# Turned answers first at a pair's end, and weight splitting one pair later between the answers, in a recurrence with two MLPs on one core

## The chip, the cores and the metric

One core of one Trainium2 chip. The metric is the device time of one launch in microseconds (us), lower is better. The engines are TensorE (PE, its weight loads are PEld), VectorE (DVE), ScalarE (ACT), GpSimd (POOL) and SyncE (SP), whose queue issues nearly all DMAs. Each runs its own instruction stream in order and waits on semaphores.

## The reference

```python
B, H, S, D = 4, 8, 768, 40
for t in range(S):                               # recurrence, a D x D state per head
    y[:, :, t] = einsum('bhd,bhde->bhe', r[t], state)
    Sa = einsum('bhde,bhe->bhd', state, a[t])
    state = state * w[t][:, :, None, :] - outer(Sa, b[t]) + outer(v[t], k[t])
x = y as (3072 tokens, 320)
h = x @ w_in;  x = (h - tanh(h)) @ w_out          # first MLP, 320 -> 2048 -> 320
p = domain_probs / (domain_probs.sum(-1) + 1e-9)
out = sum over e < 4 of p[:, e] * (relu(x @ w1[e]) @ w2[e])   # experts, 320 -> 1024 -> 320
```

## The kernel before

**Tiling.** The recurrence is solved in chunks of 128 steps (6 chunks). A unit is one chunk of four heads; there are 48 units, taken two at a time as 24 pairs (`p` = 0 to 23, four pairs to a chunk). Inside a pair the 128 steps are four blocks of 32 (`b` = 0 to 3): TensorE makes right sides, VectorE masks them (`save_right_side`, L1184), TensorE multiplies by the inverted diagonal (`answer`, L659), ScalarE copies the answers out (`save_answer`, L965). Between these TensorE does what the pair before left over (`scores_ur` L752, `result_by_answers` L739) and what the next pair needs (`scores` L777 and L781, `natural` L805, `scores_low` L792). After pairs 7, 11, 15, 19 and 23 the first MLP of the chunk before runs (`up` L895, `down` L904), the last one after all; then the experts.

**Pair end on TensorE, in order.** `natural(p+1, 0)`, `scores(p+1, 1)`, `state_by_answers(p)`, `natural(p+1, 1)`, `scores_low(p+1)`, `turn_answers(p)`. The two `natural`, `turn_answers` and `turn_state` share one PSUM bank and so wait for ScalarE's copy of the one before (`save_natural` L995, `save_turned_answers` L978). The next pair begins with `right_sides` (L632, L635), the first late diagonal (`diagonal`, L612), and `scores_ur(p)`, which waits for three things: the turned answers (L978), `save_low` (ScalarE, L983) and the rest of the low scores (ScalarE L988 up to pair 4, VectorE's `save_low_rest` L1210 from pair 5).

**Preparing later units.** In each pair up to 18 two later units are prepared: VectorE scans the decays (L1114) and inverts them (L1120 whole, L1125 in halves), GpSimd's `scale` (L1351, L1354) forms the operands, TensorE makes their diagonals, ScalarE copies those into `ld` (`save_diagonal`, L960). GpSimd ends a pair with `decay_state` (L1365), which waits for VectorE's `update_state` (L1193).

**Weight pieces.** The first MLP's weights come in 8 pieces through two slots. `PIECE_PLAN` loads piece 0 in pair 2, 1 and 2 in pair 3, 3 and 4 in pair 4, 5 in pair 5, 6 in pair 6 and 7 in pair 7; slot 0 holds pieces 0, 1, 3, 6 and slot 1 holds 2, 4, 5, 7. ScalarE's `weight_hi` (L1004, L1006, L1008) rounds a piece, GpSimd's `weight_lo` (L1376, L1380, L1384) takes the remainder and counts in `wi_lo`, four to a piece. Pieces 0 to 5 are split at the end of the pair that loads them, 6 and 7 in the first MLP. A piece may be loaded into its slot only when the one before it there has its remainder. SP's queue within a pair, shortened:

```python
early_loads(p)            # v natural (p+1), kb (p+2), store of the late unit of pair p-1
load_raw(...); load_r(p + 2); load_raw(...)
store_operands(...); store_tokens(p - 1); load_decays(p + 1)
if p == TOKENS_IN: load_tokens(0)         # waits wi_lo >= 16
for i, _ in pieces_in(p): raw_piece(i)    # waits wi_lo >= 4 * (piece before in the slot + 1)
load_a(p + 2); load_v(p + 2)
```

The operands `load_a(p + 2)` and `load_v(p + 2)` are read by `scores(p + 2, 0)`, which TensorE does in pair p + 1 between the answers of blocks 1 and 2.

Of the kernel before, what the change touches and what calls it, by code (L numbers as in the profile page):

```python
# [26 lines left out]
C = 128  # L27
# [29 lines left out]
FIRST = 10  # L57
# [52 lines left out]
def pieces_split_in(p):  # L110

    return [i for i, _ in PIECE_PLAN.get(p, []) if i < PIECES - 2]


def pieces_in(p):
# [14 lines left out]
def diagonals_before(p):  # L130

    return FIRST + sum(len(prepared_in(k)) for k in range(p - 1)) + (2 if p in (1, 2) else 0)
# [61 lines left out]
def recurrence_and_first_mlp(nc, outer, sem, pairs, ident, kbaw, rvt, vn, w_in, w_out, scratch, turned, middle, ex):  # L194
# [120 lines left out]
    def in_mlp(p):  # L315

        return prepared_in(p) if p >= 0 and drained(p) else []
# [280 lines left out]
    def _(pe):  # L598
        def diagonal(i):

            b_made, a_made = made_kb(i), made_a(i)
            o = diagonal_of(i)
            pe.wait_ge(scaled, 2 * (i + 1))
            if i in late_diagonals:
                pe.wait_ge(ut_saved, (i - FIRST) // 2 + 1)
            elif i >= FIRST:
                pe.wait_ge(lt_saved, i)
            elif i >= 2:
                pe.wait_ge(lt_saved, i - 1)
            for b in range(NB):  # L610
                for h, q, s in heads:
                    mm = pe.matmul(o[block_of(h), block_of(b)], b_made[rows(s), 1, q, block_of(b)],  # L612
                                   a_made[rows(s), q, block_of(b)], start=True, stop=True)
            mm.then_inc(lt_full, 1)
# [46 lines left out]

        def turn_state(p):

            if p:
                pe.wait_ge(ut_saved, p)
                if in_mlp(p - 1):
                    pe.wait_ge(lt_saved, diagonals_before(p + 1))
            else:
                pe.wait_ge(kbn_saved[1], 1)
            for j in range(2):  # L670
                g = 2 * (p % PPC) + j
                for q in range(2):
                    k = 2 * j + q
                    mm = pe.transpose(turn_bank[0:PR, k * PR:(k + 1) * PR], st[:, g, q, :], ident[0:PR, 0:PR])
            mm.then_inc(sn_full, 1)

        def turn_answers(p):
            if p + 1 < NP:
                pe.wait_ge(kbn_saved[1], p + 2)
            else:  # L680
                pe.wait_ge(sn_saved, p + 1)
            for j in range(2):
                pe.wait_ge(un_saved[j], NB * (p + 1))
                for q in range(2):
                    k = 2 * j + q
                    mm = pe.transpose(turn_bank[0:PR, k * C:(k + 1) * C], un[:, j, q, 0:PR], ident[:])
            mm.then_inc(ut_full, 1)
# [13 lines left out]
        def state_by_answers(p):  # L701
            for j in range(2):
                pe.wait_ge(un_saved[j], NB * (p + 1))
                for q in range(2):
                    for s in range(2):
                        mm = pe.matmul(state_bank[cols(s), state_part(j, q)], kbn[:, p % 2, j, 1, q, cols(s)],
                                       un[:, j, q, rows(s)], start=False, stop=j == 1 and q == 1)
            mm.then_inc(st_full, 1)
# [76 lines left out]
        def scores_low(p):  # L785

            pe.wait_ge(sc_saved[1], p + 1)
            for j in range(2):
                for q in range(2):
                    k = 2 * j + q  # L790
                    for s in range(2):
                        mm = pe.matmul(score_pair[0:LOW, s, k * LOW:(k + 1) * LOW], kb[rows(s), p % 2, j, 1, q, 0:LOW],  # L792
                                       at[rows(s), p % 2, j, q, BLK:C], start=True, stop=True)
            mm.then_inc(low_full, 1)

        def natural(p, j):

            if j:
                pe.wait_ge(kbn_saved[0], p + 1)
            elif p:  # L800
                pe.wait_ge(sn_saved, p)
            for a in range(2):
                for q in range(2):
                    k = 2 * a + q
                    mm = pe.transpose(turn_bank[:, k * PR:(k + 1) * PR], kb[:, p % 2, j, a, q, :], ident[0:PR, 0:PR])  # L805
            mm.then_inc(kbn_full[j], 1)
# [17 lines left out]
        def pair(p):  # L824
            after_mlp = p > 0 and drained(p - 1)
            prepared = [] if after_mlp else first_diagonals(p)
            late = last_diagonals(p)
            more = p + 1 < NP
            if not after_mlp:
                right_sides(p, 0, 0)  # L830
            right_sides(p, 1, 0)
            if after_mlp:
                pe.wait_ge(x2_saved_v, 2 * (p // PPC - 1))
                pe.wait_ge(x2_saved_a, 2 * (p // PPC - 1))
            if p:
                pe.wait_ge(st_read, p)
            for i in prepared[:1]:
                diagonal(i)
            if p and not after_mlp:
                scores_ur(p - 1)  # L840
            answer(p, 0, 0)
            answer(p, 1, 0)
            right_sides(p, 0, 1)
            right_sides(p, 1, 1)
            turn_state(p)
            for i in prepared[1:2]:
                diagonal(i)
            right_side_rest(p, 0, 1)
            right_side_rest(p, 1, 1)
            if p > 2:  # L850
                state_by_values(p)
            answer(p, 0, 1)
            answer(p, 1, 1)
            if p and not after_mlp:
                result_by_answers(p - 1)
            right_sides(p, 0, 2)
            right_sides(p, 1, 2)
            right_side_rest(p, 0, 2)
            right_side_rest(p, 1, 2)
            if more:  # L860
                scores(p + 1, 0)
            answer(p, 0, 2)
            answer(p, 1, 2)
            result_by_keys(p)
            for i in late[:1]:
                diagonal(i)
            right_sides(p, 0, 3)
            right_sides(p, 1, 3)
            right_side_rest(p, 0, 3)
            right_side_rest(p, 1, 3)  # L870
            result_by_state(p)
            for i in late[1:]:
                diagonal(i)
            if p <= 2:
                state_by_values(p)
            answer(p, 0, 3)
            answer(p, 1, 3)
            if more:
                natural(p + 1, 0)
                scores(p + 1, 1)  # L880
            state_by_answers(p)
            if more:
                natural(p + 1, 1)
                scores_low(p + 1)
            turn_answers(p)

        passes = [(HI0, HI0), (HI0, LO0), (LO0, HI0), (HI1, HI1), (HI1, LO1), (LO1, HI1), (ST2, ST2), (ST2, LO2)]

# [65 lines left out]
    def _(act):  # L954
# [81 lines left out]
        def pair(p):  # L1036
            prepared = [] if p and drained(p - 1) else first_diagonals(p)
            for i in prepared[:1]:
                save_diagonal(i)
            save_answer(p, 0, 0)  # L1040
            save_answer(p, 1, 0)
            save_turned_state(p)
            for i in prepared[1:]:
                save_diagonal(i)
            for b in range(1, NB):
                save_answer(p, 0, b)
                save_answer(p, 1, b)
                if b == 2:
                    for i in last_diagonals(p):
                        save_diagonal(i)  # L1050
            if p + 1 < NP:
                save_natural(p + 1, 0)
                save_natural(p + 1, 1)
            if p + 1 < NP:
                save_low(p + 1)
            save_turned_answers(p)
            if tokens_turned_in(p) is not None:
                tokens_hi(tokens_turned_in(p))
            for i in pieces_split_in(p):
                weight_hi(i)  # L1060

        def tanh(c, f):
            k = c * NF1 + f
# [41 lines left out]
    def _(dve):  # L1105
# [13 lines left out]
            dve.wait_ge(scanned, 2 * (i + 1))  # L1119
            dve.reciprocal(w, lam_i[:, :, 1:C + 1]).then_inc(inverted, 1)  # L1120

        def invert_half(i, q):
            w, _, _, lam_i = parts(i)
            dve.wait_ge(scanned, 2 * (i + 1))
            ins = dve.reciprocal(w[:, q, :], lam_i[:, q, 1:C + 1])  # L1125
            if q == 1:
                ins.then_inc(inverted, 1)

        def prepare(i):
# [125 lines left out]
        def pair(p):  # L1255
# [39 lines left out]
            if p + 1 < NP:  # L1295
                mask_scores(p + 1, 0)
            if p > 1 and i:
                invert_half(i[1], 0)
            some(3)
            if p + 1 < NP:  # L1300
                mask_scores(p + 1, 1)
# [1 line left out]
                prepare(i[3])  # L1303
            update_state(p)
            if p > 1 and i:
                invert_half(i[1], 1)
            if PPC < p + 1 < NP:
                save_low_rest(p + 1)

# [36 lines left out]
    def _(pool):  # L1346
# [81 lines left out]

        def pair(p):
            made_here = prepared_in(p)  # L1430
            for i in made_here:
                scale(i)
            decay_state(p)
            if tokens_turned_in(p) is not None:
                tokens_lo(tokens_turned_in(p))
            for i in pieces_split_in(p):
                weight_lo(i)

        def mlp(c, last):
            if c < 0:  # L1440
# [338 lines left out]
```

## Time and profile before

| | us |
|---|---|
| median of 3 runs (1575.66 to 1582.25) | 1577.67 |
| the profiled execution's own time | 1579.84 |
| its span, first to last instruction | 1578.1 |
| TensorE busy | 1467.6 |
| VectorE busy | 822.9 |
| ScalarE busy | 403.7 |
| GpSimd busy | 367.6 |

Times inside the trace are counted from the span's start. Pair 4 ends and pair 5 begins near 178 us, pair 6 begins near 201 us, pair 7 near 221 us; the first MLP of chunk 0 starts at 237 us; the last pair ends near 736 us and the experts follow. "Waited" below is an engine's idle time before an instruction, with what ended it.

### The profile page before, as it was taken

To read this page: it belongs to the slowest core of one execution; us is meant where nothing else is said; L and a number is where in the kernel's file an instruction comes from. 1 tells how busy PE (TensorE), PEld (TensorE's weight loads), DVE (VectorE), ACT (ScalarE), POOL (GpSimd) and SP (SyncE) were. 2 spreads that over 40 slices of the span, in tenths; PEclk is the share of its full clock that TensorE was granted. 3 is DMA by queue.
4 is the path that set the end of the run, shared out by engine and by line. 5 is a ranking of instruction groups with operands and counts; after the bars stand their busy time and mean duration, and the time that the engine had idled before them with its cause. 6 is when DMAs were issued, how large, how long until landed. Compare 5 with 4: busy or idle time off the path is not lost.

```text
span 1578.1 us, 37807 instructions
## 1 busy us (share of the span) xinstructions
PE 1467.6 (93%) x15888; PEld 1280.9 (81%) x15888; DVE 822.9 (52%) x1448; ACT 403.7 (26%) x824; POOL 367.6 (23%) x313
## 2 busy tenths in 40 slices
PE   3388889999999999999969999999999999999998
PEld 3366678778878978977958988999999999999997
DVE  8868678788778786943213333333333333333333
ACT  1132433333333333333323221111111111111111
POOL 6111545243333331311325202020010202020000
PEclk9967799999999999999989999999999999999999
DMA  7354782174165064030030311001010101000011
GB/s 193 80 142 127 190 216 81 56 189 105 37 171 141 1 174 105 1 89 20 1 108 1 104 54 37 0 0 37 0 37 0 37 0 37 0 0 0 0 50 50
DMA packets 85708, 105.29 MB, mean 67 GB/s; under 512 B 13331, under 2 KB 65555, under 8 KB 85579
## 3 DMA queue, kind: packets, MB, share of 16 engines
q1 hardware_dynamic: 84226, 102.75, 24.3%
q8 instruction: 101, 1.65, 0.5%
q10 hardware_dynamic: 1352, 0.66, 0.2%
q14 instruction: 29, 0.23, 0.1%
HBM read 74.24 MB, written 29.13 MB: 66 GB/s over the span
## 4 chain that ended last, share of the span: by engine, by line
PE 81%; DVE 11%; issue 2%; ACT 2%; DMA 1%; POOL 1%; SPq 1%; POOLq 1%; DVEq 0%; ACTq 0%
PE banks L1609 22%; PE banks L1619 21%; PE banks L895 10%; PE banks L904 9%; DVE tmp L1162 2%; PE banks L659 2%; DVE ld L1159 2%; PE banks L777 2%; DVE nvmak L1219 2%; PE banks L739 2%; PE banks L752 2%; PE banks L722 1%; PE banks L731 1%; PE banks L781 1%; PE banks L632 1%
## 5 line engine op out<-in xcount | busy, mean ns | idle before, releaser
L1609 PE MATMUL banks<-x2t,u 128*128 (+1 forms) x1536 | 376.7, 392 | 0.0
L1619 PE MATMUL banks<-u,hid 128*128 128x320 f32 x2304 | 362.5, 309 | 0.0
L1619 PEld LDWEIGHTS banks<-u,hid 128*128 128x128 f32 x2304 | 349.8, 188 | 13.1 <-issue 0.9
L1713 DVE SCALAR_TENSOR_TENSOR hid<-banks,hid 128x512 fp32r<-128x512 f32 x192 | 132.9, 692 | 404.4 <-ACT hid L1699 404.4
L1609 PEld LDWEIGHTS banks<-x2t,u 128*128 128x128 f32 x1536 | 282.5, 188 | 52.6
L1699 ACT ACTIVATE hid<-banks 128x512 fp32r<-128x512 f32 x192 | 114.7, 597 | 564.9 <-PE banks L1609 564.9
L895 PE MATMUL banks<-xt,wi 128*128 128x512 f32 x768 | 195.7, 399 | 14.6 <-POOL xt L1396 13.6
L904 PE MATMUL banks<-wo,hid 128*128 128x320 f32 x1152 | 183.5, 310 | 2.0 <-POOL hid L1401 1.6
L904 PEld LDWEIGHTS banks<-wo,hid 128*128 128x128 f32 x1152 | 174.5, 188 | 10.8 <-POOL hid L1401 3.9
L895 PEld LDWEIGHTS banks<-xt,wi 128*128 128x128 f32 x768 | 141.3, 190 | 43.3 <-POOL xt L1396 13.9
L1401 POOL TENSOR_TENSOR hid<-shared,hid 128x512 fp32r<-128x512 f32 x96 | 124.4, 1296 | 210.9 <-ACT hid L1074 210.9
L1312 DVE TENSOR_TENSOR shared<-banks,shared 128x512 f32<-128x512 f32 x96 | 66.1, 688 | 115.5 <-ACT shared L1067 115.1
L1660 POOL CAST u<-raw 128x1024 fp32r<-128x1024 f32 x7 | 7.3, 1038 | 475.2 <-PE banks L1619 462.6
L1067 ACT ACTIVATE shared<-banks 128x512 f32<-128x512 f32 x96 | 57.5, 599 | 218.6 <-PE banks L895 208.4
L1735 DVE SCALAR_TENSOR_TENSOR acc<-banks,pn,acc 128x320 f32 x168 | 80.9, 545 | 52.6 <-PE banks L1619 52.6
L965 ACT ACTIVATE un<-banks 32x160 f32<-32x160 f32 x192 | 56.5, 294 | 190.0 <-PE banks L659 187.6
L1184 DVE TENSOR_TENSOR rhs<-banks,own 128x160 f32<-128x160 f32 x192 | 53.6, 318 | 89.7 <-PE banks L649 76.6
L1351 POOL TENSOR_TENSOR made<-made 104x512 f32<-104x512 f32 x38 | 48.4, 1273 | 193.1 <-DVE made L1125 131.5
L1159 DVE TENSOR_TENSOR ld<-ld,tmp 128x31 f32<-128x31 f32 (+15 forms) x186 | 90.4, 486 | 5.5
L659 PE MATMUL banks<-rhs,tt 128*32 128x160 f32 x384 | 54.4, 347 | 33.1 <-DVE rhs L1184 30.2
L1162 DVE TENSOR_TENSOR tmp<-tt,ld 128x31 f32<-128x31 f32 (+15 forms) x155 | 76.2, 492 | 4.5
L1219 DVE TENSOR_TENSOR nvmak<-banks,upper 128x1024 f32<-128x1024 f32 x48 | 58.6, 1220 | 20.0 <-PE banks L781 20.0
(129 smaller groups left out, 1526.9 us busy)
## 6 DMA issues: line engine op xcount, KB each, us to landing
scaled_operands<-made SPq DMA_DIRECT2D x76, 192.4 KB, 3.8
kb<-scaled_operands SPq DMA_DIRECT2D x44, 192.0 KB, 3.6
made<-kbaw SPq DMA_DIRECT2D x38, 192.0 KB
made<-kbaw SPq DMA_DIRECT2D x41, 144.0 KB
raw<-w SPq DMA_DIRECT2D x8, 640.0 KB, 5.7
lam<-scaled_operands SPq DMA_DIRECT2D x44, 96.8 KB, 3.1
at<-scaled_operands SPq DMA_DIRECT2D x44, 96.0 KB, 3.0
raw<-w SPq DMA_DIRECT2D x8, 512.0 KB, 4.0
```

The source lines that it names most:

```text
L659: pe.matmul(answer_bank[answer_rows(j, b), 0:GH * HD], tt[:, :, NB * g + b], rhs[:, j, :, :].rearrange("p h d -> p (h d)"), start=True, st ...
L895: mm = pe.matmul(solve_bank(f % 2), wi[:, w, part], xt[:, x, :], start=(n == 0), stop=(n == 7))
L904: mm = pe.matmul(down_bank[t][:, 0:D], hid[:, f % HIDS, h, part], wo[:, w, f, :], start=(f == 0 and n == 0), stop=(f == NF1 - 1 and n == 2))
L1159: ins = dve.tensor_tensor(out=ti[:, j + 1:, 0:ncol], in0=ti[:, j + 1:, 0:ncol], in1=t, op=ALU.subtract)
L1162: ins = dve.tensor_tensor(out=t, in0=bc(lu[:, j + 1:, j:j + 1], [128, nr, ncol]), in1=bc(ti[:, j:j + 1, 0:ncol], [128, nr, ncol]), op=ALU. ...
L1219: dve.tensor_tensor(out=nvmak[:, j, :, :, :, :].rearrange("p s a q t -> p s (a q) t"), in0=score_pair[:, :, :].rearrange("p s (k t) -> p s ...
L1401: pool.tensor_tensor(out=hid[:, f % HIDS, 1, :], in0=gap[:, f % 2, :], in1=hid[:, f % HIDS, 0, :].bitcast(F32), op=ALU.subtract).then_inc( ...
L1609: mm = pe.matmul(self.p_up[f][:], self.u1[:, par, w, f * 128:(f + 1) * 128], self.xt[:, bass.ds(n, 1), x, :].rearrange("p o t -> p (o t)") ...
L1619: mm = pe.matmul(self.p_dn[t][:, 0:D], self.hid[:, f, h, t * 128:(t + 1) * 128], self.u2[:, par, w, f, :], start=(f == 0 and i == 0), stop ...
L1699: act.activation(ex.hid[:, f, 0, :], ex.p_up[f][:], ACT.Relu).then_inc(ex.e_hi, 1)
L1713: dve.scalar_tensor_tensor(out=ex.hid[:, f, 1, :], in0=ex.p_up[f][:], scalar=0.0, in1=ex.hid[:, f, 0, :].bitcast(F32), op0=ALU.max, op1=AL ...
L1735: dve.scalar_tensor_tensor(out=a, in0=ex.p_dn[t][:, 0:D], scalar=ex.pn[:, bass.ds(n * BATCH + t, 1), bass.ds(e, 1)] .rearrange("p o e -> p ...
```

## The change

At a pair's end `turn_answers` moves ahead of `state_by_answers`, and `natural(p+1, 1)` goes behind `scores_low(p+1)`; ScalarE's copies follow that order, and the waits on the shared bank are exchanged accordingly. VectorE inverts the second unit's second half in two quarters: one before `mask_scores(p+1, 1)`, the other after `update_state`. The splitting of pieces 0 to 5 moves from the end of the pair that loads them into the next pair: ScalarE rounds one after the answers of block 1 and one after those of block 2, GpSimd takes the first's remainder between its two scalings and the second's only in front of the first scaling of the pair after. Tokens of chunk 0 are split in pair 6 in place of pair 5's end.

```diff
+def weights_between(p):
+    pieces = pieces_split_in(p - 1)
+    return (pieces[:1], pieces[1:]) if p != TOKENS_IN + 1 else ([], pieces)
...
             if i in late_diagonals:
-                pe.wait_ge(ut_saved, (i - FIRST) // 2 + 1)
+                pe.wait_ge(kbn_saved[1], (i - FIRST) // 2 + 2)
...
         def turn_state(p):
-            if p:
-                pe.wait_ge(ut_saved, p)
-                if in_mlp(p - 1):
-                    pe.wait_ge(lt_saved, diagonals_before(p + 1))
-            else:
-                pe.wait_ge(kbn_saved[1], 1)
+            pe.wait_ge(kbn_saved[1], p + 1)
+            if p and in_mlp(p - 1):
+                pe.wait_ge(lt_saved, diagonals_before(p + 1))
...
         def turn_answers(p):
             if p + 1 < NP:
-                pe.wait_ge(kbn_saved[1], p + 2)
+                pe.wait_ge(kbn_saved[0], p + 2)
...
         def natural(p, j):
-            if j:
-                pe.wait_ge(kbn_saved[0], p + 1)
+            if j and p:
+                pe.wait_ge(ut_saved, p)
+            elif j:
+                pe.wait_ge(kbn_saved[0], 1)
...
+            turn_answers(p)
             state_by_answers(p)
             if more:
+                scores_low(p + 1)
                 natural(p + 1, 1)
-                scores_low(p + 1)
-            turn_answers(p)
...
                 save_answer(p, 1, b)
+                if b == 1 and p == TOKENS_IN + 1:
+                    tokens_hi(0)
+                if b < 3:
+                    for i in weights_between(p)[b - 1]:
+                        weight_hi(i)
...
                 save_natural(p + 1, 0)
-                save_natural(p + 1, 1)
+            save_turned_answers(p)
             if p + 1 < NP:
                 save_low(p + 1)
-            save_turned_answers(p)
-            if tokens_turned_in(p) is not None:
+                save_natural(p + 1, 1)
+            if tokens_turned_in(p) is not None and p != TOKENS_IN:
                 tokens_hi(tokens_turned_in(p))
-            for i in pieces_split_in(p):
-                weight_hi(i)
...
-        def invert_half(i, q):
-            w, _, _, lam_i = parts(i)
+        def invert_part(i, q, first, last):
+            w, lam_i = parts(i)[0], made_lam(i)
             dve.wait_ge(scanned, 2 * (i + 1))
-            ins = dve.reciprocal(w[:, q, :], lam_i[:, q, 1:C + 1])
-            if q == 1:
+            ins = dve.reciprocal(w[:, q, first:last], lam_i[:, q, 1 + first:1 + last])
+            if q == 1 and last == C:
...
             if p > 1 and i:
-                invert_half(i[1], 0)
+                invert_part(i[1], 0, 0, C)
+                invert_part(i[1], 1, 0, C // 2)
...
             update_state(p)
             if p > 1 and i:
-                invert_half(i[1], 1)
+                invert_part(i[1], 1, C // 2, C)
...
             made_here = prepared_in(p)
-            for i in made_here:
+            for i in weights_between(p - 1)[1]:
+                weight_lo(i)
+            for i in made_here[:1]:
+                scale(i)
+            if p == TOKENS_IN + 1:
+                tokens_lo(0)
+            for i in weights_between(p)[0]:
+                weight_lo(i)
+            for i in made_here[1:]:
                 scale(i)
             decay_state(p)
-            if tokens_turned_in(p) is not None:
+            if tokens_turned_in(p) is not None and p != TOKENS_IN:
                 tokens_lo(tokens_turned_in(p))
-            for i in pieces_split_in(p):
-                weight_lo(i)
```

## Rows read from the trace of the kernel before

**Rows 1.** The page's first part: busy time, share and instructions of each engine.
```profile
PE 1467.6 (93%) x15888; PEld 1280.9 (81%) x15888; DVE 822.9 (52%) x1448; ACT 403.7 (26%) x824; POOL 367.6 (23%) x313
```
**Rows 2.** What line L752 (`scores_ur`) waited for: us in total, times.
```profile
  DVE low L1210: 5.7, 12
```
**Rows 3.** TensorE's timeline at a steady boundary, pair 9 to 10: start, us, instruction.
```profile
349.63 0.46 PE L612 MATMUL banks<-made 40*32 40x32 f32 x32
350.57 1.16 PE L752 MATMUL banks<-rt,shared 40*128 40x128 f32 x16 [0.48 <-DVE low L1210]
...
356.49 0.72 PE L777 MATMUL banks<-rt,vt 40*128 40x128 f32 x8
```
**Rows 4.** VectorE's timeline around the same boundary.
```profile
346.50 1.23 DVE L1219 TENSOR_TENSOR nvmak<-banks,upper 128x1024 f32<-128x1024 f32 x1 [0.56 <-PE banks L781]
...
348.32 0.95 DVE L1125 RECIPROCAL made<-made 104x128 f32<-104x128 f32 x1
...
354.09 1.74 DVE L1120 RECIPROCAL made<-made 104x256 f32<-104x256 f32 x1
```
**Rows 5.** Timelines of ScalarE and TensorE early in pairs 5 and 6.
```profile
183.94 0.63 ACT L1004 ACTIVATE wi<-spare 128x512 fp32r<-128x512 f32 x1 [2.11 <-DMA spare<-w_out]
...
185.81 0.68 PE L612 MATMUL banks<-made 40*32 40x32 f32 x32 [4.18 <-ACT ld L960]
...
206.95 0.46 PE L612 MATMUL banks<-made 40*32 40x32 f32 x32 [2.70 <-ACT ld L960]
```
**Rows 6.** Busy time and granted clock while pair 5 resumes: us, PE, PEld, DVE, ACT, POOL, PEclk, DMA, GB/s.
```profile
185.80:192.60 6.80, 6.77 (x148) 5.46 (x148) 3.34 (x7) 1.62 (x6) 4.67 (x5) 0.57 0.72 203
```
**Rows 7.** Timelines of ScalarE and TensorE where pair 2 begins.
```profile
109.75 0.97 ACT L988 ACTIVATE low<-banks 32x512 f32<-32x512 f32 x2
...
111.44 2.08 PE L752 MATMUL banks<-rt,shared 40*128 40x128 f32 x16 [0.85 <-ACT shared L978]
```
**Rows 8.** Timelines of VectorE and TensorE at a late boundary, nothing left to prepare.
```profile
705.47 1.12 DVE L1210 COPY low<-banks 32x512 f32<-32x512 f32 x2 [0.46 <-PE banks L792]
...
706.85 1.16 PE L752 MATMUL banks<-rt,shared 40*128 40x128 f32 x16 [0.42 <-ACT shared L978]
```
**Rows 9.** VectorE's timeline in pair 3, inverse steps with and without GpSimd busy.
```profile
132.31 0.43 DVE L1162 TENSOR_TENSOR tmp<-shared,ld 128x256 f32<-128x256 f32 x1
...
133.23 1.40 DVE L1162 TENSOR_TENSOR tmp<-shared,ld 128x255 f32<-128x255 f32 x1
```
**Rows 10.** GpSimd's timeline: the last remainder of the first piece split after pair 4.
```profile
183.55 1.54 POOL L1384 TENSOR_TENSOR wo<-spare,wo 128x640 fp32r<-128x640 f32 x1 [0.22 <-issue]
```
**Rows 11.** SP's queue: piece 4's load, `load_v(6)`, the raw operands of unit 21.
```profile
176.46 0.47 SPq L495 DMA_DIRECT2D spare<-w_in  x1
...
179.81 1.46 SPq L283 DMA_DIRECT2D vt<-rvt  x4
...
185.46 0.45 SPq L266 DMA_DIRECT2D made<-kbaw  x1
```
**Rows 12.** SP's last issue of a unit's raw operands, and VectorE's scan waiting for them.
```profile
226.39 1.05 SPq L266 DMA_DIRECT2D made<-kbaw  x1
...
230.51 0.74 DVE L1114 TENSOR_TENSOR_SCAN made<-made 104x128 f32<-104x128 f32 x2 [1.00 <-DMA made<-kbaw]
```
**Rows 13.** Timelines of TensorE and VectorE in pairs 5 and 6: `scores_ur`, `scores(p+1, 0)`, `save_right_side(·, 3)`.
```profile
179.25 1.16 PE L752 MATMUL banks<-rt,shared 40*128 40x128 f32 x16 [0.47 <-DVE low L1210]
...
191.47 0.76 PE L777 MATMUL banks<-rt,vt 40*128 40x128 f32 x8
...
194.69 0.56 DVE L1184 TENSOR_TENSOR rhs<-banks,own 128x160 f32<-128x160 f32 x2 [1.41 <-PE banks L649]
...
201.85 1.16 PE L752 MATMUL banks<-rt,shared 40*128 40x128 f32 x16 [0.47 <-DVE low L1210]
...
212.16 0.72 PE L777 MATMUL banks<-rt,vt 40*128 40x128 f32 x8
...
215.34 0.56 DVE L1184 TENSOR_TENSOR rhs<-banks,own 128x160 f32<-128x160 f32 x2 [1.34 <-PE banks L649]
```

## Prediction

> **What bounds the kernel now.** I read the page first: TensorE is busy 1467.6 us of the span [rows 1], so only time in which TensorE waits, or runs at its lower clock, can be gained. Next I asked what the lines at a pair's boundary waited for. `scores_ur` waited 12 times for VectorE's low scores, 5.7 us in all [rows 2]. The timeline of one such boundary shows how: TensorE is done with the diagonal at 350.09 and begins `scores_ur` at 350.57 [rows 3]; VectorE meanwhile comes down mask, state update, half a reciprocal of 0.95, low scores [rows 4]. After that TensorE has no further wait until the pair's end. Last I looked for large waits. There are two, both early in a pair that follows a splitting of weights: 4.18 us in pair 5 and 2.70 in pair 6, each ended by ScalarE's `save_diagonal`; in front of it ScalarE stood in `weight_hi`, waiting for the piece's DMA, 2.11 us before the second piece alone [rows 5]. Behind the first of these waits the granted clock is 0.57 for 6.8 us, nearly all of it the 1.2 GHz level [rows 6].
>
> **Turned answers first.** On TensorE the swap of `turn_answers` and `natural(p+1, 1)` moves equal amounts of work; its sum is 0. What it changes is which copy ends last. At the start of pair 2 `scores_ur` waited 0.85 for the turned answers and began at 111.44, while ScalarE's low scores ended at 110.72 [rows 7]. With these as the last, it begins near 110.84: -0.6. The same at the starts of pairs 1, 3 and 4 gives nothing: pair 1 waits for the state update, and through pair 3 to the start of pair 4 VectorE's inverse steps run without a gap and set the time. At the last three boundaries inside a chunk (pairs 20 to 23) VectorE's low scores end at 706.59 and become the last, against 706.85 less the usual 0.1 to 0.15 from release to start [rows 8]: -0.15 each, -0.5 together. At the boundaries before an MLP `up` covers the wait: 0.
>
> **Reciprocal in parts.** 256 columns take 1.74 and 128 take 0.95 [rows 4]; on that line 64 take 0.55. The first quarter goes into the 0.56 that VectorE idles before `mask_scores(p+1, 1)` [rows 4] and is hidden by it, with nothing to spare; without that cover it would cost 0.55. The rest is 0.55 in place of 0.95, so the low scores end 0.40 sooner. The wait is 0.48 [rows 3], so all 0.40 arrives: twelve boundaries, -4.8. The bounds: 0, if the state update now comes late because `state_by_answers` is one place further back (it would end just as the mask does), and -5.7, the whole wait.
>
> **Splitting between the answers, ScalarE.** A piece takes about 1.5 us of ScalarE and falls between two answers, where it idles 2.4 us or more; pieces are loaded by then. Both waits of [rows 5] go. By itself that is -4.18 and -2.70, and the lower clock after them.
>
> **Remainders on GpSimd.** Piece 0's moves from the start of pair 3 to its middle, behind the first `scale`. It overlaps the same chain of inverse steps: one of them took 1.40 with GpSimd busy against 0.43 for its neighbour [rows 9]. I count three such hits, 2.7 us, before and as many after: 0, between -2.7 and +1. The Trainium skill (SBUF — State Buffer, "SBUF: two separate sides") says that the port pair of VectorE and GpSimd is an exclusive lock for a whole instruction; the rows agree, and by that rule too the sum stays 0, since the remainder meets such steps in either place.
>
> **Remainders and SP's queue.** Here I part from the gain. Piece 2's remainder now comes in pair 5, behind pair 4's `decay_state`. But `raw_piece(4)` stands in SP's queue of pair 4 and needs piece 2's remainder (`wi_lo` 12); behind it stand `load_a(6)`, `load_v(6)` and all of SP's pair 5. Step by step: the place of the remainder is that of the first piece split after pair 4 before, which ended at 183.55 + 1.54 = 185.09 [rows 10]. Everything starts 1.0 earlier (0.6 and 0.4 above): 184.1. From `raw_piece(4)` at 176.46 to the last issue of `load_v(6)` at 181.27 SP took 4.81 [rows 11]: 188.9. From a last issue's end (227.44) to the landing that released a scan (230.51) is 3.07 [rows 12]: v is there at 192.0. `scores(6, 0)` needs it. Unhindered, it would come 5.92 behind `scores_ur` [rows 3], at 178.25 + 5.92 = 184.2; so a wait of 7.8 takes the place of 4.18, and it ends 0.5 later than the 191.47 of before [rows 13]. The skill's DMA: Bandwidth & Descriptors ("Anatomy of one DMA") states that a semaphore wait happens on the issuing sequencer before dispatch; its fixed cost of about 2.0 us in place of my 3.07 would make the wait 1 us shorter, as an estimate.
>
> What is late next: unit 21's raw operands, 4.64 of issues behind `load_v` (181.27 to 185.91) [rows 11], issued by 193.5, landed by 196.6, scanned by 197.6, and `save_right_side(5, 3)` is behind the scan on VectorE. On TensorE the way from `scores` to that same point was 3.2 at full clock (194.69 - 191.47) [rows 13] and is up to 6.4 at half, which the clock after a wait suggests [rows 6]: 198.4. I take 198.2, +3.5 against 194.69. Pair 6 then begins 0.4 less late, at 205.0 (+3.1).
>
> Pair 6 repeats it: `raw_piece(5)` needs piece 4's remainder (`wi_lo` 20), which is done 5.84 behind `scores_ur` (185.09 - 179.25) [rows 10, 13], at 210.8; v(7) issued by 215.6, landed at 218.7 against 212.16; the block 3 right sides at 224.9, between 224.3 (raw operands of unit 23) and 225.1 (half clock), against 215.34 [rows 13]: +9.6. At pair 7 -0.4: +9.2. In pair 7 I work out 3 us to spare for `load_v(8)`, and `raw_piece(7)` holds back only loads that a whole MLP covers. The remaining moves (tokens split in pair 6, waits on the bank) hide under the same stretch: 0.
>
> **Sum.** +9.2 at pair 7, which has 0.6 and three of the twelve 0.4 in it; then nine boundaries of -0.4 (-3.6) and -0.5: +5.1. The profiled execution took 1579.84, so 1584.9; it was 2.2 over the median, so I predict 1577.67 + 5.1 = 1582.8. A measurement here tells about 0.5%, 7.9 us, from no change: bounds 1569.8 and 1585.6.
>
> **Rivals.**
> 1. *The queue's wait hardly matters* and the design works: -1.0 (starts), -4.18 and -2.70, the lower clock after them (from the diagonal to `scores` 5.66 and 5.21 in place of 3.6 in the steady pair [rows 3, 5, 13], -3.7), -0.8, -4.1 (later boundaries): -16.5, 1561. For it: the waits removed are the largest there are. Against: it needs v(6) by 184.2, and the code lets SP issue it only after 184.1. It decides if `scores(6, 0)` comes before about 186. Chance 0.13.
> 2. *The lower clock holds on, or the lateness reaches pair 7.* A wait of 7.8 is longer than any before it; if the half clock covers all of the rest of pairs 5 and 6 (some 7 us of work each) that adds 3 each; `load_v(8)` late adds up to 3. +8 to +14, 1586 to 1592. Chance 0.27.
> 3. *The quarter reciprocals give nothing*, as the new wait (mask or state update) eats 0.4 at each boundary: +4.8 on the sum, 1587.6. Against it stands the 0.56 of idle. Chance 0.08.
> 4. The forecast as summed, 1577 to 1588: 0.52.
>
> Of the forecast about a tenth lies above 1585.6. So faster by over 0.5%: 0.13; within: 0.48; slower: 0.39. The range that leaves out rival 1 and the far end of 2 is 1573 to 1592.
>
> **What would show it.** Right: `scores(6, 0)` and `scores(7, 0)` have idle time of some 7 us each with a DMA or nothing named as releaser; SP's L495 in pair 4's second half waits 8 to 9 us for GpSimd's L1384; no wait of L612 on L960 in pairs 5 and 6; `scores_ur` waits under 0.1 us at steady boundaries; scans L1114 in pairs 5 and 6 wait for `made<-kbaw`; the first MLP starts 9 us later than 237. Wrong: L777 without idle, or steady boundaries that still wait 0.4.

## The result, and the profile after

The changed kernel took 1585.99 us, median of 7 runs (1583.67 to 1589.81), beside 1577.67 for the kernel before (1575.66 to 1582.25): a ratio of 1.0054, 95% interval 1.0043 to 1.0065. It is 8.3 us slower; the forecast was 5.1 slower, 1582.8, and the range of 1573 to 1592 holds it. The profiled execution of after has a span of 1584.3, against 1578.1 before. Of some 130 executions in this study two lay far off all others (1639.46 of run 1 and 5149.86 of the kernel before), and they are left out of ratios and ranges.

The page of after, first part. The busy times are those of [rows 1] within 1.7 us: no engine got more work.

```profile
span 1584.3 us, 37823 instructions
...
PE 1466.7 (93%) x15888; PEld 1279.6 (81%) x15888; DVE 823.4 (52%) x1464; ACT 405.4 (26%) x824; POOL 367.5 (23%) x313
```

In the new code `scores_ur` is L755, `scores(p+1, 0)` L780, `scores_low` L795, `answer` L665, `save_right_side` L1192, the scan L1122, `save_low_rest` L1218, `weight_lo`'s last part L1393; on SP, `raw_piece` begins at L501, `load_v` is L289 and the raw operands are L270 to L272. TensorE's timeline from pair 5 to the first MLP shows what became of [rows 5] and [rows 13].

```profile
170.87 1.16 PE L755 MATMUL banks<-rt,shared 40*128 40x128 f32 x16 [0.19 <-DVE low L1218]
...
183.85 1.22 PE L780 MATMUL banks<-rt,vt 40*128 40x128 f32 x8 [7.11 <-issue]
...
191.51 0.71 PE L665 MATMUL banks<-rhs,tt 128*32 128x160 f32 x4 [0.56 <-DVE rhs L1192]
...
197.79 1.16 PE L755 MATMUL banks<-rt,shared 40*128 40x128 f32 x16 [0.18 <-DVE low L1218]
...
211.31 1.23 PE L780 MATMUL banks<-rt,vt 40*128 40x128 f32 x8 [7.65 <-issue]
...
224.26 1.16 PE L755 MATMUL banks<-rt,shared 40*128 40x128 f32 x16 [0.18 <-DVE low L1218]
...
236.39 0.71 PE L665 MATMUL banks<-rhs,tt 128*32 128x160 f32 x4 [2.00 <-DVE rhs L1192]
```

The two waits for ScalarE's `save_diagonal`, 4.18 and 2.70, are gone. In their place `scores(6, 0)` waits 7.11 and `scores(7, 0)` 7.65, with nothing named as releaser ("issue"). Pairs 5 to 6 and 6 to 7 take 26.92 and 26.47 between their `scores_ur`, against 22.60 and 20.66 before. The releaser is read one queue further back. First the line of the waits of SP's queue up to 320 us (waiting line, what it waited for, us in total, times, longest), then GpSimd's timeline of the remainders of pieces 2, 3 and 4, then SP's queue.

```profile
SPq L501 <- POOL wo L1393: 15.6, 3, 8.9
```
```profile
175.19 1.56 POOL L1393 TENSOR_TENSOR wo<-spare,wo 128x640 fp32r<-128x640 f32 x1 [0.22 <-issue]
...
181.14 1.53 POOL L1393 TENSOR_TENSOR wo<-spare,wo 128x640 fp32r<-128x640 f32 x1 [0.22 <-issue]
...
202.12 1.55 POOL L1393 TENSOR_TENSOR wo<-spare,wo 128x640 fp32r<-128x640 f32 x1 [0.22 <-issue]
```
```profile
167.28 0.59 SPq L504 DMA_DIRECT2D spare<-w_out  x1
...
176.77 0.37 SPq L501 DMA_DIRECT2D spare<-w_in  x1
...
180.03 1.46 SPq L289 DMA_DIRECT2D vt<-rvt  x4
...
185.37 0.43 SPq L272 DMA_DIRECT2D made<-kbaw  x1
...
203.70 0.40 SPq L501 DMA_DIRECT2D spare<-w_in  x1
...
207.43 1.47 SPq L289 DMA_DIRECT2D vt<-rvt  x4
...
212.63 0.43 SPq L272 DMA_DIRECT2D made<-kbaw  x1
```

Piece 2's remainder ends at 175.19 + 1.56 = 176.75, and at 176.77 SP issues piece 4; it had stood since 167.87. `load_v(6)` is behind it and is issued by 181.49; 2.36 later `scores(6, 0)` begins. Pair 6 repeats it: 203.67, 203.70, 208.90, 211.31. Later in the queue stand the raw operands of the units that the scans wait for. VectorE's timeline of after, three scans in pairs 5, 6 and 7 (of before only the third had waited, 1.00 [rows 12]):

```profile
190.50 0.74 DVE L1122 TENSOR_TENSOR_SCAN made<-made 104x128 f32<-104x128 f32 x2 [12.62 <-DMA made<-kbaw]
...
216.97 0.74 DVE L1122 TENSOR_TENSOR_SCAN made<-made 104x128 f32<-104x128 f32 x2 [12.17 <-DMA made<-kbaw]
...
235.38 0.74 DVE L1122 TENSOR_TENSOR_SCAN made<-made 104x128 f32<-104x128 f32 x2 [4.12 <-DMA made<-kbaw]
```

Windows of after, TensorE's granted clock (PEclk) behind the first wait and around pair 7's end:

```profile
184.00:188.00 4.00, 4.00 (x34) 3.29 (x36) 0.00 (x0) 1.31 (x4) 0.00 (x0) 0.50 0.98 280
...
239.50:249.70 10.20, 10.20 (x67) 8.12 (x68) 4.89 (x8) 2.52 (x4) 2.80 (x3) 0.56 0.94 224
```

At the steady boundary the wait fell from 0.48 [rows 3] to 0.18, and at `scores_low` from 0.23 to 0.16. TensorE's timeline of after:

```profile
356.09 0.92 PE L795 MATMUL banks<-at,kb 40*96 40x96 f32 x16 [0.16 <-DVE nvmak L1227]
...
358.52 1.16 PE L755 MATMUL banks<-rt,shared 40*128 40x128 f32 x16 [0.18 <-DVE low L1218]
```

The starts of `scores_ur` in both traces, after less before: pair 1 -1.0, pair 5 -8.4, pair 6 -4.1, pair 7 +1.8, pair 8 +8.1, pair 9 +8.2, pair 24 (the end) +7.0. So everything that makes after slower happens from pair 5 to pair 8: 16.4 us in these traces (16.9 if the repeat of before, run 5, is taken in place of the first trace). The -8.4 in front of it is mostly not the change's; the experiments show that.

### The profile page after: what moved, and what is told of

The parts are those of the page before. It is cut to its first block, busy times and chain, and to the rows that moved or that the text cites. A ratio compares the mean times of both kernels' runs of the same rounds, so it can differ in the third digit from the quotient of the medians.

```text
span 1584.3 us, 37823 instructions
## 1 busy us (share of the span) xinstructions
PE 1466.7 (93%) x15888; PEld 1279.6 (81%) x15888; DVE 823.4 (52%) x1464; ACT 405.4 (26%) x824; POOL 367.5 (23%) x313
## 4 chain that ended last, share of the span: by engine, by line
PE 79%; DVE 10%; issue 5%; POOL 2%; POOLq 1%; SPq 1%; DMA 1%; ACT 1%; DVEq 0%; ACTq 0%
PE banks L1624 22%; PE banks L1634 21%; PE banks L900 10%; PE banks L909 9%; PE banks L665 2%; DVE tmp L1170 2%; DVE ld L1167 2%; DVE nvmak L1227 2%; PE banks L780 2%; PE banks L755 1%; PE banks L742 1%; PE banks L725 1%; PE banks L734 1%; PE banks L784 1%; PE banks L638 1%
## 5 line engine op out<-in xcount | busy, mean ns | idle before, releaser
L1192 DVE TENSOR_TENSOR rhs<-banks,own 128x160 f32<-128x160 f32 x192 | 53.4, 317 | 73.0 <-PE banks L655 62.1
L665 PE MATMUL banks<-rhs,tt 128*32 128x160 f32 x384 | 54.7, 345 | 38.1 <-DVE rhs L1192 35.1
```

The costliest lines, as they stand in the source:

```text
L665: pe.matmul(answer_bank[answer_rows(j, b), 0:GH * HD], tt[:, :, NB * g + b], rhs[:, j, :, :].rearrange("p h d -> p (h d)"), start=True, st ...
```

## Experiments

Ratios are to the kernel before, run on the same chip in the same rounds, with 95% intervals.

**1. The second remainder taken in its own pair.** GpSimd takes both remainders between its two scalings, so SP's wait for piece 2's ends early; all else is as in after.

```diff
-            for i in weights_between(p - 1)[1]:
-                weight_lo(i)
             for i in made_here[:1]:
                 scale(i)
...
-            for i in weights_between(p)[0]:
+            for i in weights_between(p)[0] + weights_between(p)[1]:
                 weight_lo(i)
```

> Theory A (SP's queue stands behind the second piece's remainder): with both remainders between GpSimd's two scalings of the same pair, wi_lo 12 is reached near 169 us instead of 182.7 in the changed kernel's trace, before pair 4 ends. The waits of 7.1 and 7.7 us of TensorE in front of scores(6, 0) and scores(7, 0) fall to under 1 us. Pairs 5 to 7 took 76.4 us from scores_ur to scores_ur (170.87 to 247.31) against 49 for three steady pairs; raw operands still land late, so I expect 8 to 20 us of these 27 back: 1564 to 1578, faster than both kernels or level with the one before. Theory B (the later waits come from the splits standing between the answers on ScalarE and GpSimd, not from the queue): the same work stands there, so 1583 to 1589 as in the changed kernel.

Measured: 1574.88 (1570.21 to 1576.91), ratio 0.9974 (0.9961 to 0.9987). The waits at L780 are gone and the kernel is faster than before, so the late second remainder is what costs after its 8.3 us. (The 182.7 in the expectation is the end of piece 3's remainder. The one that SP waits for, piece 2's, ended at 176.75 in after, 5.88 behind pair 5's `scores_ur`; here it ends at 171.63, which is 2.13 ahead of it.) The gain is smaller than the design promises: in this trace TensorE still waits once, 3.86 at `answer`, for a right side behind a scan that waited 5.08 for its operands, and 20.5 us at about half clock follow (timelines of TensorE and VectorE, and a window).

```profile
187.76 0.98 PE L665 MATMUL banks<-rhs,tt 128*32 128x160 f32 x4 [3.86 <-DVE rhs L1192]
```
```profile
185.86 1.63 DVE L1122 TENSOR_TENSOR_SCAN made<-made 104x128 f32<-104x128 f32 x2 [5.08 <-DMA made<-kbaw]
```
```profile
188.40:208.90 20.50, 20.50 (x339) 16.47 (x338) 12.72 (x21) 6.94 (x16) 7.55 (x7) 0.53 0.94 232
```

**2. Only the two boundary parts.** Turned answers first and the reciprocal in quarters, with the weights split as before.

```diff
                 save_answer(p, 1, b)
-                if b == 1 and p == TOKENS_IN + 1:
-                    tokens_hi(0)
-                if b < 3:
-                    for i in weights_between(p)[b - 1]:
-                        weight_hi(i)
...
+            for i in pieces_split_in(p):
+                weight_hi(i)
...
-            for i in weights_between(p - 1)[1]:
-                weight_lo(i)
...
             decay_state(p)
...
+            for i in pieces_split_in(p):
+                weight_lo(i)
```

> The changed kernel with the old splitting of weights and tokens, so only the turned answers first and the reciprocal in parts. Theory A: the waits at scores(6, 0) and scores(7, 0) are gone, the waits of 4.2 and 2.7 us on ScalarE's diagonals in pairs 5 and 6 are back; the boundary waits stay at 0.2 (from 0.48). 12 boundaries by 0.36 and about 1 at the others: 5 us under the kernel before, 1572 to 1574. Theory B (the order of the turned answers costs as much as it gives): 1577 to 1582.

Measured: 1571.84 (1570.52 to 1574.24), ratio 0.9959 (0.9942 to 0.9975). The waits for `save_diagonal` are back (3.25 and 3.22), and still this is some 14 us faster than after. Beside run 1 it says more: with the second remainder out of the way the new splitting is worth nothing that can be told (0.9974 against 0.9959).

**3. Only the new splitting**, on the kernel before.

```diff
                 save_answer(p, 1, b)
...
+                if b < 3:
+                    for i in weights_between(p)[b - 1]:
+                        weight_hi(i)
...
+            for i in weights_between(p - 1)[1]:
+                weight_lo(i)
+            for i in made_here[:1]:
+                scale(i)
...
+            for i in weights_between(p)[0]:
+                weight_lo(i)
+            for i in made_here[1:]:
                 scale(i)
```

> The kernel before with only the new splitting. Theory A: it keeps both waits of 7 to 8 us and loses the 5 us of the boundaries: 1588 to 1592. If the two parts work together in some other way (the earlier turned answers bring the queue's wait about), it is level with the kernel before, 1575 to 1580.

Measured: 1589.36 (1586.55 to 1590.74), ratio 1.0068 (1.0052 to 1.0085), as theory A had it: the new splitting alone brings the loss. Its two waits are those of after, on TensorE's timeline:

```profile
187.82 1.22 PE L783 MATMUL banks<-rt,vt 40*128 40x128 f32 x8 [7.35 <-issue]
...
215.63 1.22 PE L783 MATMUL banks<-rt,vt 40*128 40x128 f32 x8 [7.90 <-issue]
```

**4. SP's queue reordered.** In after, the loads of a and v go ahead of the weight piece, so that they don't stand behind its wait.

```diff
-            for i, _ in pieces_in(p):
-                raw_piece(i)
             if p + 2 < NP:
                 load_a(p + 2)
                 load_v(p + 2)
+            for i, _ in pieces_in(p):
+                raw_piece(i)
```

> The changed kernel with load_a(p + 2) and load_v(p + 2) ahead of raw_piece in SP's queue. Theory A: the waits in front of scores(6, 0) and scores(7, 0) vanish, but the raw operands of units 21 and 23 still stand behind the piece, so VectorE's scan waits and with it save_right_side(p, 3): that point comes 16 to 17 us behind scores_ur in place of 20.3, some 3.5 us less in each of pairs 5 and 6, 1577 to 1582. Theory B: no change, 1583 to 1589. If v alone was the matter: over 12 us less, under 1574.

Measured: 1586.05 (1582.93 to 1599.71), ratio 1.0067 (1.0038 to 1.0095). I had missed: no gain. The wait at L780 is gone, as I said; but the raw operands still stand behind the piece, and most of the wait moved to them. Timelines of TensorE and VectorE, and SP's queue, of this run:

```profile
196.57 0.98 PE L665 MATMUL banks<-rhs,tt 128*32 128x160 f32 x4 [8.04 <-DVE rhs L1192]
...
223.49 0.98 PE L665 MATMUL banks<-rhs,tt 128*32 128x160 f32 x4 [3.60 <-DVE rhs L1192]
```
```profile
195.56 0.74 DVE L1122 TENSOR_TENSOR_SCAN made<-made 104x128 f32<-104x128 f32 x2 [10.16 <-DMA made<-kbaw]
```
```profile
184.30 0.37 SPq L501 DMA_DIRECT2D spare<-w_in  x1
...
191.66 0.42 SPq L272 DMA_DIRECT2D made<-kbaw  x1
```

And TensorE's clock was lower. Windows of the same stretch of this run, of after, and of a repeat of before (run 5):

```profile
184.00:240.00 56.00, 44.31 (x798) 35.15 (x787) 29.09 (x48) 16.79 (x39) 23.99 (x22) 0.63 0.70 189
```
```profile
184.00:240.00 56.00, 44.44 (x959) 35.77 (x960) 29.99 (x56) 17.71 (x43) 20.27 (x18) 0.84 0.72 192
```
```profile
184.00:240.00 56.00, 50.35 (x1107) 40.25 (x1103) 37.72 (x66) 19.85 (x47) 23.20 (x22) 0.96 0.82 212
```

TensorE is busy as long as in after, 44.3 and 44.4, but at a mean clock of 0.63 in place of 0.84, and gets through 798 matmuls in place of 959. It isn't one execution: the mean clock of this kernel's eight runs is 0.961 to 0.972, of after's seven 0.974 to 0.977, and the slowest (1599.71) has 0.961.

**5. The kernel before once more**, one execution, for its trace.

> The kernel before once more, for its profile: is the early part of the first trace (TensorE idle 0.5 and 1.3 us with nothing named near 96 and 97 us, half clock from 100 to 121 us, pair 2 beginning at 111.4) usual? If it is the kernel's own, pair 2 begins at 111 to 112 and pair 5 at 179 to 180 again; if it is scatter, pair 2 begins at 105 to 110, as in every other kernel profiled so far (104.5 to 109.4).

Measured: 1574.05, span 1572.3. Its pairs start at 106.22 (pair 2) and 174.72 (pair 5), where the first trace of before has 111.44 and 179.25: 5 us of difference between two executions of the same code, 4.1 of it made in pair 1 (1.1 at its start, 5.2 at its end) and kept to the last pair (5.1). Its waits from pair 5 on are of the same kind as those of [rows 5] (2.80 and 3.02). Against this trace, after's pair 5 starts 3.9 earlier, not 8.4.

**6. Both roundings and both remainders one block earlier.** In after, ScalarE rounds the first piece before block 1's answers and the second after them; GpSimd takes the first remainder before its first scaling and the second behind it, in the same pair.

```diff
+            for i in weights_between(p)[0]:
+                weight_hi(i)
...
-                if b < 3:
-                    for i in weights_between(p)[b - 1]:
+                if b == 1:
+                    for i in weights_between(p)[1]:
                         weight_hi(i)
...
-            for i in weights_between(p - 1)[1]:
+            for i in weights_between(p)[0]:
                 weight_lo(i)
             for i in made_here[:1]:
                 scale(i)
...
-            for i in weights_between(p)[0]:
+            for i in weights_between(p)[1]:
                 weight_lo(i)
```

> As the first experiment, but the first piece is rounded ahead of block 1's answers and the second behind them, and the first one's remainder stands ahead of GpSimd's first scaling. Theory A (what is left over in pair 5 is the raw operands of unit 21, issued behind piece 4, which waits for piece 2's remainder): that remainder ends 2 to 3 us sooner against pair 5's begin, VectorE's wait of 5.1 us for the raw operands shrinks by as much and TensorE's 3.9 to about 1: 1570 to 1573. Rival: the copies ahead of block 1's answers delay the chain of answers, or the wait has another cause: 1575 or more.

Measured: 1570.73 (1568.76 to 1576.08), ratio 0.9968 (0.9956 to 0.9979). It beats the kernel before by 0.3% and after by 0.9% (0.9968 / 1.0054), and is level with runs 1 and 2, whose intervals overlap with its own. The time fell into the expected range, but not by the expected mechanism. Against pair 5's begin piece 2's remainder ends no sooner than in run 1 (165.79 against 168.00, 2.2 ahead; 2.1 in run 1). VectorE's wait for the raw operands is 6.45, not less than the 5.08 of run 1, and 4.40 more in pair 6. TensorE waits 2.95 and 1.26 at L780 and 1.69 at L665. SP's queue no longer waits for a remainder here, so these waits have another cause: from the last issue of `load_v(6)` (172.80) to the start of L780 it is 4.02, where after had 2.36. Timelines of TensorE and VectorE:

```profile
176.82 0.71 PE L780 MATMUL banks<-rt,vt 40*128 40x128 f32 x8 [2.95 <-issue]
```
```profile
181.45 1.02 DVE L1124 TENSOR_TENSOR_SCAN made<-made 104x128 f32<-104x128 f32 x2 [6.45 <-DMA made<-kbaw]
```

In the traces run 6 gains on run 1 in pairs 2, 4 and 5 (19.57 against 22.00, 17.08 against 19.54, 21.02 against 23.53) and loses as much in pairs 6 and 7 (23.19 against 20.01, 21.02 against 17.44), so what its change is worth by itself was not found.

**7. Only turned answers first** (run 2 without the quarters).

```diff
-                invert_part(i[1], 1, 0, C // 2)
...
-                invert_part(i[1], 1, C // 2, C)
+                invert_part(i[1], 1, 0, C)
```

> The kernel before with only the turned answers first, reciprocal in halves. Theory: at the twelve steady boundaries VectorE's low scores still end last, wait 0.4 to 0.48 as before; only the three last boundaries and those of pairs 2 and 3 gain: 1575.5 to 1577.5. Rival (the two changes of the boundary give the same 0.3 each, whichever comes first): 1572 to 1574.

Measured: 1580.93 (1575.73 to 1589.05), ratio 1.0025 (1.0007 to 1.0043): slower than before, which neither theory had. The wait at `scores_ur` grew from 0.48 to 0.59, but 0.07 of this only moved there from `scores_low`, whose wait fell from 0.23 to 0.16. The low scores end 0.04 later against the mask in front of them (3.96 behind its start, 3.92 before), and that is all a boundary loses. What the trace does show is one fall of the clock, between pairs 10 and 11, in a part (pair 9 to the last) where every other trace of this study has the full clock. TensorE's timeline, and a window:

```profile
327.48 1.87 PE L755 MATMUL banks<-rt,shared 40*128 40x128 f32 x16 [0.58 <-DVE low L1215]
...
347.82 0.38 PE L755 MATMUL banks<-rt,shared 40*128 40x128 f32 x2 [0.59 <-DVE low L1215]
```
```profile
328.00:340.00 12.00, 12.00 (x225) 9.56 (x224) 6.01 (x11) 3.00 (x10) 6.68 (x6) 0.58 0.72 188
```

That pair took 20.34 in place of 16.28. The twelve runs spread with the clock: the four at 0.976 or more took 1575.73 to 1577.01, the six at 0.972 or less 1581.04 to 1589.05. The middle of those four, 1576.6, lies 0.6 above the 1575.98 of before in the same rounds, and twelve boundaries of 0.04 are 0.5. The rest goes with the clock: before's 28 executions have 0.976 to 0.982, and eight of these twelve lie under 0.976. Why it falls more often here is not shown.

**8. Only the reciprocal in quarters**, on the kernel before.

```diff
-                invert_half(i[1], 0)
+                invert_part(i[1], 0, 0, C)
+                invert_part(i[1], 1, 0, C // 2)
...
-                invert_half(i[1], 1)
+                invert_part(i[1], 1, C // 2, C)
```

> The kernel before with only the reciprocal in parts. VectorE's low scores then end at 350.02 on the scale of the steady boundary, level with the turned answers of ScalarE (349.45 + 0.57 = 350.02), so `scores_ur` waits 0.1 in place of 0.48: twelve times 0.3 to 0.4, 1573 to 1574.5. Rival (turned answers late by as much as the low scores were): 1576 to 1578.

Measured: 1575.24 (1569.75 to 1580.08), ratio 0.9996 (0.9982 to 1.0009). Its runs lie wide, from 1569.75 at a clock of 0.982 to 1580.08 at 0.972, and by time it doesn't decide between the expectations. The trace does say that the expected mechanism came: no boundary from pair 5 to pair 19 shows a wait of `scores_ur` any more, where before nine from pair 8 on had 4.31 together. But only 1.3 to 1.4 of this reaches the last pair (pair 8 to the last 494.63, in the two traces of before 496.06 and 495.91). Part of the gain comes back as waits with a load behind them: 0.60 and 1.05 at L698, in pairs 9 and 14, for 0.33 and 0.52, and 0.82 at an `answer` in pair 15, behind a scan that waits for raw operands. Timelines of TensorE and VectorE:

```profile
475.10 0.30 PE L659 MATMUL banks<-rhs,tt 128*32 128x160 f32 x1 [0.82 <-issue]
```
```profile
474.98 0.74 DVE L1114 TENSOR_TENSOR_SCAN made<-made 104x128 f32<-104x128 f32 x2 [1.19 <-DMA made<-kbaw]
```

The rest stays open. So does why the two parts together gave -0.41% and alone +0.25% and -0.04%; what the traces show of it is that turning first needs the quarters to bring the wait at `scores_ur` to 0.18 from 0.59.

## Why the prediction was right, and where it was not

**The queue's wait: right, and the cause is shown.** Pair 5 was to grow by 4.1 and grew by 4.3; pair 6 by 6.1 and grew by 5.8 (against the repeat of before 5.8 and 5.3, so the closeness is partly luck of the trace). The waits at `scores` were to be 7.8 in pair 5 and are 7.11 and 7.65; SP's longest wait for the remainder was to be 8 to 9 and is 8.9. Run 1 takes out only the place of the second remainder and turns +0.54% into -0.26%. The term from the last issue's end to the release, 3.07 from [rows 12], was one reading used for two kinds of load. For `load_v` it was too large: 2.36 and 2.41 in pairs 5 and 6. For the raw operands it was too small in the same pairs: 190.50 - 185.80 = 4.70 and 216.97 - 213.06 = 3.91, and 235.38 - 232.39 = 2.99 in pair 7. The two errors nearly cancel in the sum of a pair. The Trainium skill (DMA: Bandwidth & Descriptors, "Anatomy of one DMA") gives about 2.0 us of fixed cost for a DMA, stated for GpSimd's software path, not SP's. The 2.36 of `load_v` lies near to it, the 4.02 in run 6 (if it is this load that L780 waits for there) does not; all these readings have a transfer in them.

**Rival 1 (the design works)** lost at its own condition: it needed v(6) about 8 us behind `scores_ur` (186 against 178.25), and it came 12.98 behind (183.85 - 170.87). Run 1 shows what it would have been worth: not 16.5 us but some 4, and no more than run 2 has without the new splitting. Even when the queue's long wait is gone TensorE still waits 3.86 there, and 20.5 us at about half clock follow.

**The lateness that reaches pair 7: the step that failed.** I gave pair 7 nothing (the -0.4 stands at its start), since I had "3 us to spare for `load_v(8)`". v(8) was in time; the raw operands of unit 25 were not. SP came out of pair 6 late and stayed so: their last issue ended at 232.39, 4.95 after the 227.44 of before, while the pair itself had begun only 1.75 later.

```profile
229.94 1.52 SPq L270 DMA_DIRECT2D made<-kbaw  x1
...
231.97 0.42 SPq L272 DMA_DIRECT2D made<-kbaw  x1
```

The scan waited 4.12, TensorE 2.00 at 236.39, and the half clock above (239.5 to 249.7) took the rest: pair 7 grew by 6.3, from 16.74 to 23.05. How much is the clock's part varies: in run 3, with the same splitting, the scan waited 3.17 and TensorE 1.05, the clock stayed full (1.00 from 240 to 248), and pair 7 took 18.30. This is rival 2's mechanism, which I had given a chance of 0.27 and a size of up to 3. Its other half, a half clock over the rest of pairs 5 and 6, did not come.

**Early pairs.** I had -1.0 at pair 5; the traces show -8.4 against the first trace of before and -3.9 against its repeat. 4.5 of it is the scatter between executions that run 5 measured; of the 2.9 that is left beyond my -1.0 no run shows the cause. Moving piece 0's remainder cost nothing, as forecast: from pair 3 to pair 4 27.50 against 27.31, and 27.67 in the repeat.

**Steady boundaries: right in kind, too large in sum.** Each wait shrank by 0.30 and `scores_low`'s by 0.07, near the 0.40 forecast; the sign "under 0.1" was missed (0.18), as was the first MLP's start, 243.62 against 237.24, so 6.4 later and not 9. But from pair 8 to the last only 1.1 us came of it (8.1 to 7.0), where I had 4.1 (nine boundaries, and 0.5). A place where it goes is seen in pair 9, the first behind an MLP: the gain returns as a wait at `state_by_values` (L701, before L698), 0.68 for 0.33, and in pair 17 `scores` (L780) waits 0.72 that before did not have. Run 8 shows the same kind. TensorE's timeline and SP's queue of after:

```profile
329.96 0.42 PE L701 MATMUL banks<-vnat,kbn 128*64 128x40 f32 x8 [0.68 <-issue]
```
```profile
323.51 0.39 SPq L292 DMA_DIRECT2D vnat<-vn  x1
```

It begins 6.45 after the issue of v natural, and before it was 6.46 (314.98 to 321.44); in the five other traces that wait there it is 6.33 to 6.93. So most likely that load sets it; no run moved it. At the last boundaries, 0.42 [rows 8] became 0.38 and not 0.27, since the low scores ended as late as the turned answers had.

**Terms that cancelled.** In the traces: 7.4 too early at pair 5, 0.1 less in pairs 5 and 6, 6.3 too late out of pair 7, and 3.1 of boundary gain not had (-7.4 - 0.1 + 6.3 + 3.1 = +1.9); the sum at the last pair was +7.0 where I had +5.1. The forecast's size is thus partly luck: a term that I put at nothing (pair 7) and one that hardly arrived (the boundaries) were offset by an early part that is mostly scatter. The mechanism of the queue's wait is not luck. The two parts measured apart (-0.41% and +0.68%) add up to +0.27%, and together they gave +0.54%; the difference is at the edge of what the intervals allow.

## What to carry to other kernels

When work that frees a buffer is put off, look for the load that needs the buffer and then read everything that stands behind it in the in-order queue: here 8.9 us of wait for a weight piece held up operands that had nothing to do with it, for two pairs and more. Moving some of those loads ahead only hands the wait to the next ones (run 4); freeing the buffer sooner takes it away (runs 1 and 6), though what is left is then no faster than the kernel without the new splitting (run 2). And a part of a change that looks harmless alone may need its partner (run 7), so measure the parts apart before dropping one.

## What the runs showed of the hardware

- **The clock can fall in a stretch without any long wait, in some executions of a kernel more often than in those of its neighbour.** In run 7's trace a 12 us stretch behind a wait of 0.58 ran at a granted clock of 0.58, most of it the 1.2 GHz level, and its pair took 4 us more. The Trainium skill (TensorE: Matmul & The Clock Gate, "A second HAM failure mode: psum-queue depth-cycling") tells of a clock that goes back and forth under frequent micro-idles. The trace neither confirms nor excludes this as the cause: the eight other waits of that size from pair 9 on had no such stretch behind them, and a boundary's two waits come to 0.75 in run 7, 0.71 before and 0.34 in after.
- **Half clock can last far longer than the wait in front of it, and by no fixed time**: 20.5 us at 0.53 after a wait of 3.86 (run 1), 16 us at 0.50 (204 to 220) soon after one of 1.69 (run 6), and a clock of 0.63 over 56 us with waits of 8.04 and 3.60 (run 4), as against 0.84 over the same stretch of after with 7.11 and 7.65, where the clock is full again from 192 to 204. The longer waits did not bring the lower clock; what decides was not found.
- **Two executions of one kernel drew apart by 4.1 us in pair 1 alone**, and stood 4.5 to 6.0 apart from there on. A difference between two single traces early in this kernel says little below that size.
